# Attention, Fourier mixing and a gated convolution layer in fp32: two more products rounded for cheaper matmuls, another choice of added middle taps, and VectorE steps in another order

## The chip, the cores and the metric

The kernel runs on one core of one Trainium2 chip. The metric is the device time of one execution in microseconds (us), as a median over runs. All times below are in us.

## The reference, cut to what matters

Three layers follow each other on 4 batches of 1088 tokens with 128 channels. The first is a linear attention with product features, the second a Fourier mix over tokens and channels, a normalisation and a two-matmul layer (512 hidden channels), the third, where the change lies, is this one (1024 hidden channels, a convolution over tokens with three taps for each channel):

```python
def _moe2_ref(x, w_in, conv_w, w_out):
    h = np.maximum(x @ w_in, 0.0)
    hp = np.concatenate([zeros, h, zeros], axis=1)      # one token each side
    for k in range(3):
        conv_out += conv_w[k][None, None, :] * hp[:, k:k + S, :]
    gate = 1.0 / (1.0 + np.exp(-conv_out))
    return h * gate @ w_out
```

## The kernel before, in words

Channels lie on the 128 partitions, tokens in the free dimension. The second layer ("layer 1" in the change's words: normalised rows, w1, w2) is cut into ten units of four row tiles; a unit has four slots (one for each 128 of its 512 hidden channels), so there are 40 slots and two to finish them. The third layer is cut into 32 chunks, chunk i being batch i // 8 and the hidden channels i % 8 of 128. From chunk 0 on, both are interleaved by PACES: slots 23 to 41 are spread over the steps 0 to 22, in two places in each step (slots_a and slots_b).

In a step i TensorE does hidden(i) (L671, three matmuls of 364 tokens, each as three passes of a rounded number split into a high and a low half, L612), perhaps normed_transposes, slots, and project(n) (L686) of a chunk that lies LAGS steps back. A chunk runs through these instructions:

- relu (L894, ScalarE, three pieces) writes h2(i), a ring of HIDDENS = 5 buffers; relu(i) waits for product(i - 5).
- The left and the middle tap. Three ways: left_tap (L1177, VectorE) does both in one instruction. For chunks in ADDED, the left tap is a scaled copy on ScalarE (left_copy, L902) or, for those in SCALED, on VectorE (left_scaled, L1184), and the middle tap is an accumulating DMA from POOL's queue (add_middle, L474). An added chunk is "late": its right tap and all behind it come one step later.
- right_tap (L1190, VectorE), sigmoid (L911, ScalarE), product (L1199, VectorE; chunks 30 and 31 in three parts).
- project: plain, one fp32 matmul for each third of the tokens, which the trace shows as two records (L707), or, for chunks in CAST, "rounded": a DMA from POOL's queue casts the product to a rounded fp32 (cast_product, L483, three buffers, gate_hi, so that cast n waits for the project of the chunk three casts before), product_low (L1206, VectorE) takes what is left over, and the matmul is three passes.

Each engine works its list in order, written out by hand in the step loops: ScalarE's at L933, VectorE's at L1221, POOL's at L491, TensorE's at L754. Layer 1's low halves on VectorE are hidden_low (L1117), mixed_low (L1124) and normed_low (L1109); mixed_rows (L1072) adds the Fourier mix to a row set, moments and late_rows normalise. Slots 19 and 21 hold the normed_low of places 6 and 7, and the transposes of place 7 write the PSUM bank that the halves of place 6 are read from (L624). The adds and the casts alternate between two semaphores each, so that each waits for the one two before it.

The step loop of VectorE, in the order before:

```python
                for i in products_at(step):
                    product(i)
                if step + 1 in LAST_TURNS:
                    normed_low(LAST_TURNS[step + 1])
                for n in slots_a(step + 1):
                    slot(n)
                for i in rights(step):
                    right_tap(i)
```

Of the kernel before, what the change touches and what calls it, by code (L numbers as in the profile page):

```python
# [90 lines left out]
TURNS_AT = {2: 1, 6: 2, 10: 3, 14: 4, 17: 5, 19: 6, 21: 7}  # L91
# [2 lines left out]
PACES = ((0, 23), (30, 34), (46, 42))  # L94
HIDDENS = 5
VECTOR_ROWS = (8, 9)
ADDED = (4, 6, 7, 8, 9, 11, 12, 13, 15, 16, 17, 18, 20, 22, 24, 25, 26, 27, 28, 30)
CAST = (2, 4, 5, 6, 7, 11, 12, 13, 16, 17, 20, 21)
CASTS = 3
SCALED = (11, 17, 28)  # L100
ADDED_LATE, PRODUCT_AT, LOW_AT = 1, 2, 3
H2_PAD, H2_ROW = 15, 1120
GATES = 9
SPLIT_FROM = NI - 2
LAGS = ((-1, 7), (28, 6), (30, 5))
FINAL_LAG = LAGS[-1][1]
assert TQ * NJ == HALF and TT * NT == SP and TT % 2 == 0 and G1 % 2 == 0 and G1 <= 512

# [8 lines left out]
def build(nc, kT_d, qT_d, v_d, s_d, ident_d, chan_d, cos_d, sin_d, w1_d, w2_d, win_d, wout_d, cw_d, out_d):  # L117
    with ExitStack() as ctx:
# [143 lines left out]
        def bank_h1(n):  # L262
            return 2 + n % 3 if n < FIRST_SLOTS else 2
# [30 lines left out]
        def has_low(n):  # L294
            return n < LOW_UNTIL


        def products(i, t):
            return PRODUCT_ORDER.index(i) + 1 if i < SPLIT_FROM else SPLIT_FROM + NT * (i - SPLIT_FROM) + t + 1
# [5 lines left out]
        def gate(i):  # L305
            return attic[:, (i % GATES) * S:(i % GATES + 1) * S]


        def halves_free(n):

            return ((wout_done, NT * (CAST[n - CASTS] + 1)),) if n >= CASTS else ()


        def late(i):
            return ADDED_LATE if i in ADDED else 0


        COPIED = [i for i in ADDED if i not in SCALED]

        def rights(step):  # L320
            both = (step - ADDED_LATE, step) if step == NI - 1 else (step, step - ADDED_LATE)
            return [i for i in both if 0 <= i < NI and i + late(i) == step]
# [6 lines left out]
        def products_at(step):  # L329
            return [i for i in (step - PRODUCT_AT - ADDED_LATE, step - PRODUCT_AT) if 0 <= i < NI and i + PRODUCT_AT + late(i) == step]  # L330
# [18 lines left out]
        def slots_before(place):  # L349
            for (p0, n0), (p1, n1) in zip(PACES, PACES[1:]):  # L350
                if place <= p1:
                    return n0 + -(-(n1 - n0) * (place - p0) // (p1 - p0))
            return NC1 + 2
# [28 lines left out]
        def slots_b(i):  # L382
            return range(slots_before(2 * i + 1), slots_before(2 * i + 2))
# [50 lines left out]
        def _(pool):  # L434
# [39 lines left out]
            def add_middle(n, i):  # L474
                if i in SCALED:
                    pool.wait_ge(scaled, SCALED.index(i) + 1)
                else:
                    pool.wait_ge(copied, COPIED.index(i) + 1)
                if n >= 2:
                    pool.wait_ge(middle_added[n % 2], 16 * (n // 2))  # L480
                pool.dma_start(gate(i), h2(i)[:, 1:S + 1], accum_op=ALU.add).then_inc(middle_added[n % 2], 16)

            def cast_product(n, i):  # L483
                pool.wait_ge(prod_ready, products(i, 0))
                if n >= 2:
                    pool.wait_ge(cast_done[n % 2], 16 * (n // 2))
                for free, count in halves_free(n):
                    pool.wait_ge(free, count)
                pool.dma_start(gate_hi[:, n % CASTS, :], gate(i)).then_inc(cast_done[n % 2], 16)

            for step in STEPS:  # L491
                if step in ADDED:
                    add_middle(ADDED.index(step), step)
                for i in products_at(step):
                    if i in CAST:
                        cast_product(CAST.index(i), i)


        @block.tensor
        def _(pe):  # L500
# [185 lines left out]
            def project(i):  # L686
                b, c = divmod(i, C2)
                if i == 0:
                    pe.wait_ge(ld_wout, 32)
                n = CAST.index(i) if i in CAST else None  # L690
                if n == 0:
                    pe.wait_ge(wout_lo_ready, 1)
                if i in CAST:
                    pe.wait_ge(cast_done[n % 2], 16 * (n // 2 + 1))
                    pe.wait_ge(low_ready, n + 1)
                for t in range(NT):
                    if i not in CAST:
                        pe.wait_ge(prod_ready, products(i, t))
# [254 lines left out]
        def _(dve):  # L953
# [155 lines left out]
            def normed_low(r):  # L1109
                dve.wait_ge(unhi_ready, r + 1)  # L1110
                if 2 <= r < RING:
                    dve.wait_ge(w1_done, C1 * (r - 1))
                high, low = turned(r)
                dve.tensor_tensor(low, ps[:, bank_turned(r), 0:G1], high.bitcast(F32),  # L1114
                                  ALU.subtract).then_inc(unlo_ready, 1)

            def hidden_low(n):  # L1117
                dve.wait_ge(h1hi_ready, n + 1)
                if n >= 3:
                    dve.wait_ge(w2_done, n - 2)  # L1120
                dve.scalar_tensor_tensor(out=h1lo[:, n % 3, :], in0=ps[:, bank_h1(n), 0:G1], scalar=0.0,  # L1121
                                         in1=h1hi[:, n % 3, :].bitcast(F32), op0=ALU.max, op1=ALU.subtract).then_inc(h1lo_ready, 1)

            def mixed_low(r):  # L1124
                dve.wait_ge(x2hi_ready, written(r))
                for (turned, tokens), (_, high) in zip(token_views(x2lo, r), token_views(x2hi, r)):
                    dve.tensor_tensor(tokens, turned, high.bitcast(F32), ALU.subtract).then_inc(x2lo_ready, 1)  # L1127

            def slot(n):
                r, c = divmod(n, C1)  # L1130
                if n < NC1 and has_low(n):
                    hidden_low(n)
                if n in MIXED_AT:
                    mixed_rows(MIXED_AT[n])
                if c == 1 and r >= NJ:
                    mixed_low(r - 1)
                if n in MOMENTS_AT:
                    moments(MOMENTS_AT[n])
                if c == 2 and 1 <= r < NJ:
                    mixed_low(r - 1)  # L1140
                if n in TURNS_AT:
                    normed_low(TURNS_AT[n])
                if n in ROWS_AT and ROWS_AT[n] in VECTOR_ROWS:
                    late_rows(ROWS_AT[n])
# [45 lines left out]
            def right_tap(i):  # L1190
                if i in ADDED:
                    n = ADDED.index(i)
                    dve.wait_ge(middle_added[n % 2], 16 * (n // 2 + 1))
                else:
                    dve.wait_ge(left_ready, i - sum(n < i for n in ADDED) + 1)
                dve.scalar_tensor_tensor(out=gate(i), in0=h2(i)[:, 2:S + 2], scalar=ratio[:, 1, i % C2:i % C2 + 1],  # L1196
                                         in1=gate(i), op0=ALU.mult, op1=ALU.add).then_inc(conv_ready, 1)

            def product(i):  # L1199
                dve.wait_ge(gate_ready, SIGMOID_ORDER.index(i) + 1)  # L1200
                cuts = [t * TT for t in range(NT)] if i >= SPLIT_FROM else [0]
                for a, z in zip(cuts, cuts[1:] + [S]):
                    dve.tensor_tensor(gate(i)[:, a:z], h2(i)[:, 1 + a:1 + z], gate(i)[:, a:z],  # L1203
                                      ALU.mult).then_inc(prod_ready, 1)

            def product_low(n, i):  # L1206
                dve.wait_ge(cast_done[n % 2], 16 * (n // 2 + 1))
                dve.tensor_tensor(gate_lo[:, i % GATES, :], gate(i), gate_hi[:, n % CASTS, :].bitcast(F32),
                                  ALU.subtract).then_inc(low_ready, 1)
# [11 lines left out]
            for step in STEPS:  # L1221
                if step in SCALED:
                    left_scaled(step)
                elif step < NI and step not in ADDED:
                    left_tap(step)
                for i in products_at(step):
                    product(i)
                if step + 1 in LAST_TURNS:
                    normed_low(LAST_TURNS[step + 1])
                for n in slots_a(step + 1):  # L1230
                    slot(n)
                for i in rights(step):
                    right_tap(i)
                if step == 0:
                    late_rows(NR - 1)
                if step == 3:
                    wout_low()
                for n in slots_b(step + 1):
                    slot(n)
                for i in CAST:  # L1240
                    if i + LOW_AT + late(i) == step:
                        product_low(CAST.index(i), i)


def lag(i):

    return next(chunks for first, chunks in reversed(LAGS) if i >= first)

# [88 lines left out]
```

## Time and profile before

| | |
|---|---|
| median of 3 runs | 251.67 us (251.54 to 251.69) |
| the profiled execution | 252.02 us |
| its span, first to last instruction | 250.2 us |
| TensorE matmuls busy | 242.9 us, 97% |
| VectorE busy | 215.4 us, 86% |
| ScalarE busy | 170.8 us, 68% |
| granted TensorE clock | full in every slice |

The span is what the profile's times are counted in; 1.8 us of the execution lie around it. Matmuls are pipelined, so a matmul's duration is longer than the time it holds the engine, and the distance between two starts is what counts; the same holds, by a little, for VectorE and ScalarE. Idle time stands in square brackets behind an instruction, with the one that ended it.

### The profile page before, as it was taken

What the parts mean: (1) busy time and instruction counts of PE and PEld (TensorE: products, weight loads), DVE (VectorE), ACT (ScalarE), POOL (GpSimd) and SP (SyncE); (2) the same over time, 40 slices, a digit from 0 to 9 for tenths busy, and PEclk for the clock granted to TensorE, in tenths of its full rate; (3) what the DMA queues carried; (4) which work ended last, traced back from release to release, by engine and by line L of the source; (5) the groups of instructions that cost most, each with busy time, mean ns of one, the idle gap of its engine ahead of it and who ended that gap; (6) DMA issues with size and microseconds to landing.
All of it is one profiled execution on the core that took longest, in us unless ns stands there. A gap on an engine that the chain in (4) does not pass through costs nothing.

```text
span 250.2 us, 4440 instructions
## 1 busy us (share of the span) xinstructions
PE 242.9 (97%) x1558; PEld 215.1 (86%) x1558; DVE 215.4 (86%) x408; ACT 170.8 (68%) x334; POOL 53.3 (21%) x123
## 2 busy tenths in 40 slices
PE   8999999999999999998989999999999999999995
PEld 6999999999989998997978877998879879797753
DVE  0747888899998697899899999988969999989992
ACT  2452634332576566667799898999958989997852
POOL 0000000000624530665501332031421211321100
PEclk9999999999999999999999999999999999999999
DMA  6968830210000020000004799387988446997602
GB/s 194 392 243 320 344 101 3 62 40 0 3 0 0 4 84 1 3 3 3 0 0 89 186 261 217 141 165 195 262 206 158 135 134 181 280 196 157 170 3 89
DMA packets 9094, 31.41 MB, mean 126 GB/s; under 512 B 1264, under 2 KB 2032, under 8 KB 9072
## 3 DMA queue, kind: packets, MB, share of 16 engines
q0 software_dynamic: 4752, 18.35, 30.8%
q1 hardware_dynamic: 4176, 12.74, 14.1%
q8 instruction: 13, 0.21, 0.4%
q14 instruction: 9, 0.07, 0.1%
q10 hardware_dynamic: 144, 0.03, 0.1%
HBM read 10.54 MB, written 2.23 MB: 51 GB/s over the span
## 4 chain that ended last, share of the span: by engine, by line
PE 41%; DVE 11%; ACT 2%; issue 1%; ACTq 0%
PE ps L707 10%; PE ps L613 9%; PE ps L615 9%; PE ps L614 9%; PE ps L656 4%; DVE attic L1196 4%; DVE attic L1203 3%; DVE attic L1181 2%; DVE late_lo L1114 1%; PE ps L647 1%; ACT folded_room L900 1%; ACT arena L829 1%; DVE x2lo L1127 0%; ACT attic L915 0%; DVE wout_lo L1213 0%
## 5 line engine op out<-in xcount | busy, mean ns | idle before, releaser
L915 ACT ACTIVATE attic<-attic,base 128x1088 f32<-128x1088 f32 x32 | 37.9, 1204 | 4.6 <-DVE attic L1196 4.5
L707 PE MATMUL ps<-attic,wout 128*128 128x364 f32 (+1 forms) x120 | 39.1, 469 | 0.1
L613 PE MATMUL ps<-x2hi,wlo 128*128 128x364 f32 x96 | 37.2, 388 | 0.8 <-ACT folded_room L900 0.7
L707 PEld LDWEIGHTS ps<-attic,wout 128*128 128x128 f32 x120 | 22.5, 189 | 13.2 <-issue 2.1
L615 PE MATMUL ps<-x2hi,whi 128*128 128x364 f32 x96 | 31.6, 329 | 0.0
L614 PE MATMUL ps<-x2lo,whi 128*128 128x364 f32 x96 | 31.5, 328 | 0.0
L613 PEld LDWEIGHTS ps<-x2hi,wlo 128*128 128x128 f32 x96 | 18.1, 188 | 4.9 <-ACT folded_room L900 1.7
L900 ACT ACTIVATE x_room<-ps 128x364 f32<-128x364 f32 x42 | 18.3, 479 | 4.0 <-PE ps L615 3.7
L458 POOL TENSOR_SCALAR arena<-arena 109x4 f32<-109x4 f32 x10 | 2.0, 197 | 88.4 <-DVE arena L1099 88.3
L1196 DVE SCALAR_TENSOR_TENSOR attic<-x_room,ratio,attic 128x1088 f32<-128x1088 f32 x14 | 18.7, 1348 | 1.7 <-DMA attic<-x_room 1.6
L614 PEld LDWEIGHTS ps<-x2lo,whi 128*128 128x128 f32 x96 | 18.1, 188 | 2.4 <-issue 1.1
L780 ACT ACTIVATE attic<-ps 109x320 f32<-109x320 f32 (+2 forms) x16 | 6.7, 425 | 18.4 <-PE ps L528 16.1
L540 PE MATMUL ps<-attic 121*128 121x66 f32 x144 | 18.6, 270 | 0.0
L1203 DVE TENSOR_TENSOR attic<-x_room,attic 128x1088 f32<-128x1088 f32 (+2 forms) x18 | 18.1, 1035 | 0.4 <-ACT attic L915 0.4
L900 ACT ACTIVATE folded_room<-ps 128x364 f32<-128x364 f32 x36 | 15.3, 477 | 4.1 <-PE ps L615 3.9
L615 PEld LDWEIGHTS ps<-x2hi,whi 128*128 128x128 f32 x96 | 18.0, 188 | 0.0
L1121 DVE SCALAR_TENSOR_TENSOR h1lo<-ps,h1hi 128x436 fp32r<-128x436 f32 x22 | 13.2, 605 | 5.5 <-ACT h1hi L843 5.5
L540 PEld LDWEIGHTS ps<-attic 121*128 121x128 f32 x144 | 17.7, 192 | 0.0
L571 PE MATMUL ps<-arena 128*109 128x66 f32 x160 | 17.1, 260 | 0.1
L528 PE MATMUL ps<-sketch,attic 128*109 128x64 f32 (+1 forms) x152 | 17.1, 267 | 0.0
L788 ACT ACTIVATE arena<-ps 128x436 f32<-128x436 f32 x20 | 10.6, 534 | 9.3 <-PE ps L555 9.2
L528 PEld LDWEIGHTS ps<-sketch,attic 128*109 128x109 f32 (+1 forms) x152 | 16.7, 185 | 0.2
(130 smaller groups left out, 621.6 us busy)
## 6 DMA issues: line engine op xcount, KB each, us to landing
gate_hi<-attic POOLq DMA_DIRECT2D x12, 544.0 KB, 3.5
attic<-folded_room POOLq DMA_DIRECT2D x9, 544.0 KB, 5.0
attic<-x_room POOLq DMA_DIRECT2D x8, 544.0 KB, 5.3
attic<-v_d SPq DMA_DIRECT2D x4, 594.0 KB, 3.8
attic<-qT_d SPq DMA_DIRECT2D x3, 545.0 KB, 7.0
attic<-kT_d SPq DMA_DIRECT2D x3, 544.5 KB, 6.1
attic<-arena POOLq DMA_DIRECT2D x3, 544.0 KB, 5.3
out_d<-arena SPq DMA_DIRECT2D x3, 544.0 KB, 4.7
```

The source lines that it names most:

```text
L528: mm = pe.matmul(ps[0:rows, bank_kq(n), c:c + H * AB], src[:, b % 2, t * rows:(t + 1) * rows], sketch[:], start=True, stop=True)
L540: mm = pe.matmul(ps[:, KV_BANK, pair * 2 * V1:(pair + 1) * 2 * V1], kphi[:, b % 2, t, 2 * pair:2 * pair + 2, :].rearrange("p h f -> p (h f)"),
L571: mm = pe.matmul(ps[0:TQ, bank, c:c + 2 * V1], qphiT[:, 2 * t + pair, :], kvz[:, pair, :], start=True, stop=True)
L613: pe.matmul(out, lo, rhi, start=first, stop=False)
L614: pe.matmul(out, hi, rlo, start=False, stop=False)
L615: return pe.matmul(out, hi, rhi, start=False, stop=last)
L707: pe.matmul(ps[:, OUT_BANK + t, 0:z - a], wout[:, c, :], gate(i)[:, a:z], start=(c == 0), stop=(c == C2 - 1)).then_inc(wout_done, 1)
L900: act.activation(h2(i)[:, t * TT:(t + 1) * TT], ps[:, bank_p(n), 0:TT], ACT.Relu).then_inc(h2_ready, 1)
L915: act.activation(gate(i), gate(i), ACT.Sigmoid, scale=base[:, i % C2:i % C2 + 1]).then_inc(gate_ready, 1)
L1121: dve.scalar_tensor_tensor(out=h1lo[:, n % 3, :], in0=ps[:, bank_h1(n), 0:G1], scalar=0.0, in1=h1hi[:, n % 3, :].bitcast(F32), op0=ALU.max ...
L1196: dve.scalar_tensor_tensor(out=gate(i), in0=h2(i)[:, 2:S + 2], scalar=ratio[:, 1, i % C2:i % C2 + 1], in1=gate(i), op0=ALU.mult, op1=ALU.a ...
L1203: dve.tensor_tensor(gate(i)[:, a:z], h2(i)[:, 1 + a:1 + z], gate(i)[:, a:z], ALU.mult).then_inc(prod_ready, 1)
```

## The change

It does five things.

- CAST gets the chunks 3 and 8: 14 rounded projections, not 12.
- ADDED loses 8 and 27 and gets 10 (19, not 20); SCALED loses 28, which stays added and gets its scaled copy on ScalarE. 8 and 27 become left taps.
- LAGS: project stays 7 steps behind up to step 28 and is 6 behind from 29 on (before: 7, 6 from 28, 5 from 30). So the projections come in the order 21 | 22, 23 | 24 | 25 in the steps 28 to 31, and 26 to 31 behind the last step (before 21, 22 | 23 | 24, 25 | 26, and 27 to 31).
- In VectorE's step loop the right taps come ahead of the late normed_low and of slots_a; the lows of the rounded products come ahead of slots_b.
- In slot 19 the normed_low of place 6 comes ahead of mixed_rows.

```diff
-ADDED = (4, 6, 7, 8, 9, 11, 12, 13, 15, 16, 17, 18, 20, 22, 24, 25, 26, 27, 28, 30)
-CAST = (2, 4, 5, 6, 7, 11, 12, 13, 16, 17, 20, 21)
+ADDED = (4, 6, 7, 9, 10, 11, 12, 13, 15, 16, 17, 18, 20, 22, 24, 25, 26, 28, 30)
+CAST = (2, 3, 4, 5, 6, 7, 8, 11, 12, 13, 16, 17, 20, 21)
 CASTS = 3
-SCALED = (11, 17, 28)
+SCALED = (11, 17)
...
-LAGS = ((-1, 7), (28, 6), (30, 5))
+LAGS = ((-1, 7), (29, 6))
...
                 if n < NC1 and has_low(n):
                     hidden_low(n)
+                if n in TURNS_AT and n == 19:
+                    normed_low(TURNS_AT[n])
                 if n in MIXED_AT:
                     mixed_rows(MIXED_AT[n])
...
-                if n in TURNS_AT:
+                if n in TURNS_AT and not n == 19:
                     normed_low(TURNS_AT[n])
...
                 for i in products_at(step):
                     product(i)
+                for i in rights(step):
+                    right_tap(i)
                 if step + 1 in LAST_TURNS:
                     normed_low(LAST_TURNS[step + 1])
                 for n in slots_a(step + 1):
                     slot(n)
-                for i in rights(step):
-                    right_tap(i)
                 if step == 0:
                     late_rows(NR - 1)
                 if step == 3:
                     wout_low()
-                for n in slots_b(step + 1):
-                    slot(n)
                 for i in CAST:
                     if i + LOW_AT + late(i) == step:
                         product_low(CAST.index(i), i)
+                for n in slots_b(step + 1):
+                    slot(n)
```

## Rows read from the trace of the kernel before

**Rows 1.** The page's first part: busy time, share and instructions of each engine.

```profile
PE 242.9 (97%) x1558; PEld 215.1 (86%) x1558; DVE 215.4 (86%) x408; ACT 170.8 (68%) x334; POOL 53.3 (21%) x123
```

**Rows 2.** Busy by stretches: PE, PEld, DVE, ACT, POOL, then clock, DMA share, GB/s.

```profile
139.00:157.00 18.00, 17.87 (x85) 14.25 (x85) 17.27 (x18) 15.65 (x30) 5.14 (x7) 1.00 0.96 245
...
240.00:250.20 10.20, 7.29 (x24) 3.95 (x22) 5.65 (x9) 3.83 (x5) 0.00 (x0) 1.00 0.16 56
```

**Rows 3.** The chain that ended last: start, length, engine and line.

```profile
140.33 2.54 DVE attic L1196 x2
...
145.60 0.43 PE ps L613
...
152.05 1.83 PE ps L707 x6
...
235.89 0.18 PE ps L615
...
242.89 0.55 DVE attic L1203
...
243.48 3.94 PE ps L707 x12
```

**Rows 4.** TensorE's timeline: start, length, line and operation, operands, idle before.

```profile
114.82 0.56 PE L626 MATMUL ps<-ident,arena 109*128 109x109 f32 x4 [1.03 <-DVE late_lo L1114]
...
116.81 0.39 PE L613 MATMUL ps<-x2hi,wlo 128*128 128x364 f32 x1
...
147.20 0.33 PE L613 MATMUL ps<-gate_hi,wout_lo 128*128 128x364 f32 x1
...
148.68 0.36 PE L613 MATMUL ps<-late_hi,wlo 128*128 128x436 f32 x1
...
158.05 0.33 PE L613 MATMUL ps<-x2hi,wlo 128*128 128x364 f32 x1
```

**Rows 5.** VectorE's timeline.

```profile
112.74 0.48 DVE L1081 TENSOR_TENSOR arena<-ps,arena 109x130 f32<-109x130 f32 x2
...
114.08 0.60 DVE L1114 TENSOR_TENSOR late_lo<-ps,late_hi 128x436 fp32r<-128x436 f32 x1
...
115.64 0.67 DVE L1127 TENSOR_TENSOR x2lo<-ps,x2hi 128x218 fp32r<-128x218 f32 x2
...
122.56 1.12 DVE L1106 TENSOR_SCALAR arena<-x_room,arena 109x128 f32<-109x128 f32 x4 [0.65 <-POOL arena L472]
...
143.14 1.29 DVE L1208 TENSOR_TENSOR gate_lo<-attic,gate_hi 128x1088 fp32r<-128x1088 f32 x1 [0.28 <-DMA gate_hi<-attic]
...
147.28 0.74 DVE L1127 TENSOR_TENSOR x2lo<-ps,x2hi 128x218 fp32r<-128x218 f32 x3 [0.44 <-ACT x2hi L848]
...
152.86 1.29 DVE L1203 TENSOR_TENSOR attic<-x_room,attic 128x1088 f32<-128x1088 f32 x1
154.06 1.35 DVE L1196 SCALAR_TENSOR_TENSOR attic<-folded_room,ratio,attic 128x1088 f32<-128x1088 f32 x1
155.33 1.35 DVE L1181 SCALAR_TENSOR_TENSOR attic<-x_room,ratio 128x1088 f32<-128x1088 f32 x1
...
161.52 0.79 DVE L1188 TENSOR_SCALAR attic<-x_room,ratio 128x1088 f32<-128x1088 f32 x1
```

**Rows 6.** ScalarE's timeline.

```profile
112.05 1.66 ACT L829 ACTIVATE arena<-x_room,arena 109x128 f32<-109x128 f32 x4
...
145.09 1.18 ACT L900 ACTIVATE folded_room<-ps 128x364 f32<-128x364 f32 x3
```

**Rows 7.** POOL's timeline.

```profile
119.36 1.21 POOL L466 TENSOR_TENSOR arena<-arena 109x4 f32<-109x4 f32 x1
...
138.17 0.56 POOL L489 DMA_DIRECT2D gate_hi<-attic  x1 [4.13 <-DVE attic L1203]
```

**Rows 8.** The lines L489 (12 casts) and L481 (20 adds): from issue to landing.

```profile
DMA to landing us min/median/max: 2.9/3.5/5.0
...
DMA to landing us min/median/max: 4.6/5.2/7.4
```

## The prediction

> **What bounds the kernel now.** I read the page's busy shares first: TensorE's matmul side is busy 97% of the span [rows 1]. So a gain must come either from fewer or cheaper matmul instructions, or from the few places where TensorE stands still. Next the table by stretches: in 139 to 157 us VectorE is busy 17.27 of 18 us and the 16 DMA engines 96%, at the full granted clock; at the end TensorE is busy 7.29 of 10.2 us, and most of what is missing there is the tail behind its last matmul [rows 2]. Then the chain that ended last. It shows three kinds of place: a wait for VectorE before 114.8 us, a VectorE-ScalarE-TensorE hand-over up to 145.60, and from there TensorE without a break until 235.89 plus its own width; after that the last chunk's VectorE work, and TensorE again at 243.48 [rows 3]. Timelines of the single engines give the sizes:
>
> - In the gap before the transposes of place 7, TensorE sat idle for 1.03 until 114.82, waiting for the low half that VectorE finished at 114.68 [rows 4, 5].
> - At 145.60 hidden(9) follows project(1): it waited for the relu of chunk 8 that started at 145.09, itself behind two sigmoids that waited for the right taps of 5 and 4 (140.33) [rows 3, 6].
> - At the end, four plain projections of 1.83 fill 235.89 to 243.21, and product(30), from 242.89 on, lets the next start at 243.48: 0.27 lost [rows 3].
>
> I call left, right, product, low the VectorE work on a chunk (L1181, L1196, L1203, L1208). By starts in a row without idle, a product or low takes 1.20 and a tap 1.26 (152.86, 154.06, 155.33) [rows 5].
>
> **Step 1: the low half of place 6 ahead of mixed rows 9.** It now starts at 114.08, behind 1.34 of mixed rows; it will start at 112.74 and end at 113.34. The next thing the transposes need is the scaled rows, which ScalarE finishes at 112.05 + 1.66 = 113.71 [rows 5, 6]. So TensorE goes on at about 113.85, 0.97 earlier. Not all of it is kept. Nothing behind both VectorE pieces moves: their sum is the same. hidden(0), at 116.81 now, needs the second part of the low half at 115.64, done at 116.31: it starts at about 116.4, 0.4 earlier [rows 4, 5]. The mixed rows end 0.52 later, hidden by the h1 low halves, which start at 114.60 as before. From here VectorE's own queue decides up to 145.6, and its idle time there (0.65 at 122.56, and a smaller wait for the low half of place 8, which the right tap of 1, now ahead of it, fills) gives back what it can [rows 5]. I take 0.36 at 145.60; the ends are 0.1 (only the relu of chunk 0 a bit earlier) and 0.4 (all that hidden(0) has gained). The late half of place 9 starts 1.2 later, cover: its reader, slot 28, comes after hidden(6).
>
> **Step 2: chunks 3 and 8 rounded.** A plain projection is six records and 1.83; a rounded one is nine, 147.20 to 148.68 = 1.48 [rows 3, 4]. That is 0.35 less on TensorE for each, 0.70 together. VectorE gets two lows, 2.40; POOL two casts, the DMA engines two transfers. Nothing else of the dtype changes.
>
> **Step 3: the middle taps.** 8 and 27 go from a ScalarE copy and an accumulating DMA to a left tap, 10 the other way, 28 from a VectorE scaling (0.79) to a ScalarE copy. VectorE: +1.26 three steps early in the crowded stretch (chunk 8), -1.26 at 10, +0.56 net at 27/28 (1.35 - 0.79) [rows 5]. The DMA engines lose one add.
>
> **Where steps 2 and 3 meet: relu(11).** The hidden values lie in a ring of five, so relu(11) waits for product(6), and hidden(12), at 158.05 now, waits for relu(11) [rows 4]. From low(2) at 143.14 to product(6) at 152.86 VectorE now spends 9.72. After the change low(3) (1.20), left(8) (1.26) and right(8) (1.26, one step earlier, since 8 is no longer late) stand ahead of product(6) too; right(6) ahead of slot 29 fills the idle 0.44 at 147.28 [rows 5]. 9.72 + 3.72 - 0.44 = 13.00. low(2) starts at 143.14 - 0.36 = 142.78, product(6) at 155.78, ends at 157.07; relu(11) at 157.1; hidden(12) 0.51 after it, as 145.09 to 145.60 now [rows 3, 6]: 157.6, 0.45 before its place now. TensorE by itself would be 0.36 + 0.35 = 0.71 ahead. So here VectorE, not TensorE, sets the pace, and every wait in its queue before 155.8 counts in full.
>
> **The unknown: when cast 3 lands.** product(3) ends about 139.97, its cast can be issued at about 140.3, and low(3)'s turn is 143.98. Casts take 2.9 to 5.0 to land, median 3.5; the one issued at 138.17 just ahead took the 5.0 [rows 7, 8]. So the wait of low(3) lies between 0 (2.9 and 3.5) and 1.3 (5.0). A longer one isn't excluded: add(6) now comes right behind cast 3 on POOL, and adds take 4.6 to 7.4 [rows 8]. I take 4.0, nearer to the median: 0.3 of wait. The POOL queue is also held by the ring of three rounded halves: cast 5 now waits for project(2), 148.68 (its low's turn is after 154), cast 8 for project(5), with add(11) behind it; add(10) is queued behind cast 6, at about 158.3, and right(10)'s turn is 163, with a landing of 5.2 a wait of 0.5. product(9) then ends about 168.4, and relu(14), which waits for it, may start up to 169.1 before hidden(15) moves. Cost taken: 0, bounds 0 and 0.6.
>
> A row speaks against this: at 119.36 a 0.20 us POOL operation took 1.21 and ended 0.05 after VectorE's tap [rows 7]. The Trainium skill (SBUF — State Buffer, the trap "DVE blocks DMA") says that GpSimd can't write the descriptors of its DMA while certain VectorE instructions hold the port pair that both share. By that rule a cast might wait one further tap, 1.35, and the sum below would end at about +0.5; against it, the issue instruction of the cast at 138.17 took 0.56, and VectorE was busy then too, so the landing times above hold what there is of it [rows 7].
>
> **Step 4: right taps ahead of slots, lows ahead of slots, the lag.** Only slots 25, 29, 33, 37, 41 have VectorE work; the lows' move changes no order at all, the right taps' move steps 7, 17 and 21. Slot 29's low halves, needed by a transpose three records behind 148.68, about 149.3, end by 149.0 to 149.8: 0 to 0.4 of stall, taken as 0. With the lag, project(25) comes behind hidden(31): seven chunks behind it, not six, so the last hidden chunk comes 1.83 earlier and VectorE has 1.83 more for the tail, against +0.56 of step 3. The sigmoid of 26, behind the output copies on ScalarE, costs it some 0.6 by my walk through the order. product(30) then starts at 242.89 - 1.83 - 0.50 + 0.56 + 0.6 = 241.7 (0.50 is what TensorE has gained by then). Its first part, 0.55, is due at 243.21 - 0.50, so it may start up to 242.2 [rows 3]: the 0.27 wait goes, and some 0.03 more in the last split parts. Taken: 0.30, bounds 0 and 0.38.
>
> **Sum.** hidden(12): -0.45 + 0.3 = -0.15. project(8): -0.35. End: -0.30. Together -0.80. The profiled execution took 252.02 (span 250.2); it would take 251.2. It stands 0.35 above the median of the runs, 251.67, and I subtract from that: 250.9.
>
> **The rivals.**
> - Cast 3 lands as its neighbour does (5.0): -0.45 + 1.3 - 0.65 = +0.2, 251.9. For it: DMA engines at 96%, an add right behind. Against: most casts were faster. 0.22.
> - Slower: low(3) is held as adds are. Place: VectorE at 144 us, everything behind it up to relu(11). At 6.3 (between 5.2 and 7.4) the wait is 2.6: +1.5, 253.2. It decides from a landing of about 5.3 on (+0.5). The rule above pulls this way. 0.11.
> - TensorE's own limit: no cast wait, and VectorE catches up: -0.36 - 0.70 - 0.30 = -1.36, 250.3. For it: a landing of 3.5. Against: the 13.00 of VectorE work. 0.15.
> - The reorder doesn't do what it is said to: TensorE at 114 us is held by the rows from ScalarE or VectorE's queue gives nothing back, so 0.36 is 0: -0.44, 251.2. 0.10.
> - The forecast: 0.42.
>
> **The numbers.** A measurement of this kernel tells 0.2%, 0.5 us, from no change. Faster by more: forecast 0.42, limit 0.15, and 0.06 of the fourth rival: 0.63. Within: 0.22 + 0.04: 0.26. Slower: 0.11. The range 250.2 to 252.2 takes in -1.4 (limit) and +0.5 (cast landing at 5.3); it leaves out the slower rival.
>
> **What would show it.** TensorE's gap at 114.8 down to some 0.2; rounded projections at 1.48 for chunks 3 and 8; product(6) at about 156.1, VectorE waiting some 0.3 for cast 3, and hidden(12) at 157.9; a gap of some 0.5 in TensorE right before it; no wait before product(30)'s projection. The forecast is wrong if hidden(12) isn't earlier than 158.05, if low(3) waits over 1 us, or if a new wait stands behind 170 us, where I count none.

## The result, and the profile after

The changed kernel is slower: 252.71 us, median of 12 runs, against 252.01 of 12 of the kernel before on the same chip. Some executions of most kernels here, before too, take 33 us more, all of it ahead of hidden(0) where a trace shows one (e2, e4, f2, h3: hidden(0) at 149.5 to 149.8, otherwise 115.9 to 117.2), so they are left out of the table's medians and of the ratios, and the stretches of those four stand in brackets. By the 11 and 10 executions that are left the medians are 252.59 and 251.84, and the ratio is 1.0032, with a 95% interval of 1.0021 to 1.0042, so 0.8 us. The forecast was 250.9. The profiled execution took 252.48 with a span of 250.7, against 252.02 and 250.2: of the 0.8 the trace shows some 0.5.

The page's busy shares, after, answer to [rows 1]: VectorE has 3.2 us more work.

```profile
PE 243.1 (97%) x1564; PEld 216.2 (86%) x1564; DVE 218.6 (87%) x410; ACT 170.0 (68%) x334; POOL 53.7 (21%) x124
```

The table by stretches, columns as in [rows 2]:

```profile
139.00:157.00 18.00, 17.49 (x87) 14.29 (x86) 17.96 (x18) 15.51 (x27) 4.38 (x6) 1.00 0.82 218
...
240.00:250.70 10.70, 7.90 (x26) 4.58 (x25) 5.99 (x9) 3.83 (x5) 0.00 (x0) 1.00 0.14 52
```

Between 139 and 157 us VectorE is busy 17.96 of 18.00 us: nothing is left there. TensorE lost 0.38 of its 17.87.

TensorE's timeline of the changed kernel, which answers to [rows 4]:

```profile
113.82 0.59 PE L626 MATMUL ps<-ident,arena 109*128 109x109 f32 x4
...
116.88 0.40 PE L613 MATMUL ps<-x2hi,wlo 128*128 128x364 f32 x1 [0.63 <-DVE x2lo L1127]
...
149.93 0.56 PE L647 MATMUL ps<-ident,x_room 109*128 109x109 f32 x4 [0.45 <-DVE x2lo L1127]
...
170.72 0.44 PE L613 MATMUL ps<-x2hi,wlo 128*128 128x364 f32 x1 [0.51 <-ACT arena L900]
```

The gap of 1.03 at 114.82 is gone, but a gap of 0.63 stands ahead of hidden(0), which starts at 116.88, not at 116.4. And there are two new gaps: at slot 29's transposes, 149.93, and ahead of hidden(15), 170.72.

VectorE's timeline (left L1183, scaled L1190, right L1198, product L1205, low L1210), which answers to [rows 5]:

```profile
115.71 0.67 DVE L1127 TENSOR_TENSOR x2lo<-ps,x2hi 128x218 fp32r<-128x218 f32 x2
...
142.88 2.59 DVE L1210 TENSOR_TENSOR gate_lo<-attic,gate_hi 128x1088 fp32r<-128x1088 f32 x2
145.38 1.28 DVE L1205 TENSOR_TENSOR attic<-arena,attic 128x1088 f32<-128x1088 f32 x1
...
147.79 1.35 DVE L1198 SCALAR_TENSOR_TENSOR attic<-x_room,ratio,attic 128x1088 f32<-128x1088 f32 x1
149.05 0.73 DVE L1127 TENSOR_TENSOR x2lo<-ps,x2hi 128x218 fp32r<-128x218 f32 x3
...
156.01 1.28 DVE L1205 TENSOR_TENSOR attic<-x_room,attic 128x1088 f32<-128x1088 f32 x1
...
163.44 1.35 DVE L1198 SCALAR_TENSOR_TENSOR attic<-x_room,ratio,attic 128x1088 f32<-128x1088 f32 x1 [0.58 <-DMA attic<-x_room]
...
167.60 1.29 DVE L1210 TENSOR_TENSOR gate_lo<-attic,gate_hi 128x1088 fp32r<-128x1088 f32 x1 [1.43 <-DMA gate_hi<-attic]
168.81 1.28 DVE L1205 TENSOR_TENSOR attic<-arena,attic 128x1088 f32<-128x1088 f32 x1
```

The two lows at 142.88 are low(2) and low(3), with no wait. Low(8), at 167.60, waited 1.43 for its cast. The casts and adds on POOL, by the DMA-issuing instructions of L489 and L481:

```profile
157.59 0.55 POOL L489 DMA_DIRECT2D gate_hi<-attic  x1 [6.66 <-DVE attic L1205]
158.12 0.92 POOL L481 DMA_DIRECT2D attic<-x_room  x1
159.15 0.55 POOL L489 DMA_DIRECT2D gate_hi<-attic  x1
163.45 0.53 POOL L489 DMA_DIRECT2D gate_hi<-attic  x1 [3.76 <-PE ps L615]
```

These are cast 6, add 10, cast 7 and cast 8. Cast 8 is held until project(5) has read its half. The chain that ended last goes through it, and at the end it has no step of VectorE any more:

```profile
163.45 4.12 DMA gate_hi<-attic
167.60 1.29 DVE gate_lo L1210
168.90 1.21 DVE attic L1205
170.19 0.48 ACT arena L900
170.72 0.44 PE ps L613
...
235.10 12.81 PE ps L707 x42
```

**Where the time went.** I measure a stretch, from the start of the second record of hidden(9) to the end of TensorE's last matmul, since the start of the whole shifts a little from one execution to the next. Before, that is 247.42 - 145.87 = 101.55; after, 247.91 - 145.88 = 102.03. By the second records of the hidden chunks, and counted from that of hidden(9), it divides into: hidden(10) 0.68 later (slot 29's gap); project(3), between hidden(10) and hidden(11), 4.65 to 4.36, so -0.29; hidden(15) a further 0.77 later (1.16 in all; its first record is at 170.72); project(8), between hidden(15) and hidden(16), 5.04 to 4.75, so -0.29; and the end -0.39. Together +0.48. The table gives this stretch for each kernel. It is one execution each: two of the changed kernel, this one and h3, differ by 0.19, so stretches that are closer than 0.2 can't be told apart. The ratio isn't the quotient of the two medians beside it (for g2 that is 0.9973, for g3 0.9975, for h2 0.9964); differences of 0.1% are not to be read.

| kernel | what differs | median us | before, same chip | ratio (95%) | stretch us |
|---|---|---|---|---|---|
| before | | 251.84 | | 1 | 101.55 |
| changed | | 252.59 | 251.84 | 1.0032 (1.0021 to 1.0042) | 102.03 |
| e1 | right(6) behind slot 29 | 252.1, 252.83 | 251.91 | none (two runs) | 101.83 |
| e2 | chunk 8 plain | 251.75 | 251.91 | 0.9988 (0.9977 to 0.9999) | (101.34) |
| e3 | both of these | 251.50 | 251.91 | 0.9982 (0.9969 to 0.9995) | 101.10 |
| e4 | slot 19's order as before | 252.86 | 251.91 | 1.0036 (1.0024 to 1.0049) | (102.74) |
| f1 | low(8) a step later | 253.42 | 251.94 | 1.0057 (1.0035 to 1.0078) | 102.89 |
| f2 | f1 and e1 | 253.63 | 251.94 | 1.0053 (1.0028 to 1.0079) | (102.98) |
| f3 | e3, lag as before | 251.74 | 251.94 | 0.9991 (0.9977 to 1.0006) | 102.00 |
| f4 | chunk 3 plain | 251.55 | 251.94 | 0.9981 (0.9966 to 0.9995) | 100.98 |
| g1 | e1, low(8) behind slot 33 | 254.25 | 252.09 | 1.0069 (1.0048 to 1.0089) | 102.75 |
| g2 | chunks 3 and 8 plain | 251.41 | 252.09 | 0.9965 (0.9952 to 0.9978) | 101.20 |
| g3 | the kernel before, new lag | 251.45 | 252.09 | 0.9967 (0.9955 to 0.9979) | 101.15 |
| g4 | add 10 ahead of cast 6 | 252.03 | 252.09 | 0.9994 (0.9979 to 1.0008) | 101.79 |
| h1 | g4 and e1 | 251.91 | 251.96 | 0.9996 (0.9979 to 1.0013) | 101.50 |
| h2 | g4 and f4 | 251.06 | 251.96 | 0.9959 (0.9943 to 0.9975) | 100.90 |
| h3 | the changed kernel again | 252.83 | 251.96 | 1.0038 (1.0015 to 1.0060) | (101.84) |

All edits are made to the changed kernel, but for g3.

### The profile page after: what moved, and what is told of

Same layout as the page of the kernel before. It is cut to its first block, busy times and chain, and to the rows that moved or that the text cites. A ratio compares the mean times of both kernels' runs of the same rounds, so it can differ in the third digit from the quotient of the medians.

```text
span 250.7 us, 4455 instructions
## 1 busy us (share of the span) xinstructions
PE 243.1 (97%) x1564; PEld 216.2 (86%) x1564; DVE 218.6 (87%) x410; ACT 170.0 (68%) x334; POOL 53.7 (21%) x124
## 4 chain that ended last, share of the span: by engine, by line
PE 36%; DVE 14%; POOL 2%; DMA 2%; issue 1%; ACT 1%; POOLq 0%; ACTq 0%
PE ps L707 12%; PE ps L613 7%; PE ps L615 7%; PE ps L614 7%; DVE attic L1205 3%; PE ps L656 3%; DVE attic L1198 3%; DVE attic L1183 2%; DMA gate_hi<-attic 2%; DVE gate_lo L1210 2%; DVE x2lo L1127 1%; DVE late_lo L1114 1%; DVE arena L1093 1%; PE ps L647 1%; POOL arena L468 1%
## 5 line engine op out<-in xcount | busy, mean ns | idle before, releaser
L707 PE MATMUL ps<-attic,wout 128*128 128x364 f32 (+1 forms) x108 | 34.7, 468 | 0.0
L707 PEld LDWEIGHTS ps<-attic,wout 128*128 128x128 f32 x108 | 20.4, 190 | 11.7 <-issue 1.6
L1210 DVE TENSOR_TENSOR gate_lo<-attic,gate_hi 128x1088 fp32r<-128x1088 f32 x14 | 18.0, 1288 | 2.2 <-DMA gate_hi<-attic 2.1
L1198 DVE SCALAR_TENSOR_TENSOR attic<-x_room,ratio,attic 128x1088 f32<-128x1088 f32 x14 | 18.7, 1349 | 0.9 <-DMA attic<-x_room 0.8
L1205 DVE TENSOR_TENSOR attic<-x_room,attic 128x1088 f32<-128x1088 f32 (+2 forms) x18 | 18.1, 1034 | 0.4 <-ACT attic L915 0.2
L489 POOL DMA_DIRECT2D gate_hi<-attic x14 | 7.7, 549 | 44.2 <-DVE attic L1205 32.8
```

What stands on the lines that cost most here:

```text
L707: pe.matmul(ps[:, OUT_BANK + t, 0:z - a], wout[:, c, :], gate(i)[:, a:z], start=(c == 0), stop=(c == C2 - 1)).then_inc(wout_done, 1)
```

## The experiments

### The two new gaps, each undone

e1 puts right(6) back behind slot 29, as before:

```diff
-                for i in rights(step):
+                for i in rights(step) if step != 7 else ():
                     right_tap(i)
...
                 for n in slots_a(step + 1):
                     slot(n)
+                for i in rights(step) if step == 7 else ():
+                    right_tap(i)
```

> The changed kernel, but in step 7 the right tap of 6 comes behind slot 29 again, as before the change. Theory (two separate new stalls): TensorE's 0.45 us gap ahead of the transposes at 149.9 goes, hidden(10) is back near 150.6, and since cast 8 waits for project(5) it is issued 0.6 earlier too, so hidden(15) and the end come 0.6 earlier: 0.9975 of the changed kernel, about 252.1. Rival (VectorE simply has more work than fits, and sets the pace wherever it is asked): right(6), left(8) and the lows move back by the 0.44 of idle that slot 29 then costs, product(6) is at 156.4, and the end moves by less than 0.2 us.

Measured: TensorE's timeline of e1 at the two places:

```profile
149.14 0.54 PE L647 MATMUL ps<-ident,x_room 109*128 109x109 f32 x4
...
170.28 0.43 PE L613 MATMUL ps<-x2hi,wlo 128*128 128x364 f32 x1 [0.85 <-ACT arena L900]
```

So with right(6) behind slot 29 the gap there goes, and hidden(10) comes 0.65 earlier (counted from hidden(9)). But the gap ahead of hidden(15) grew from 0.51 to 0.85, and at hidden(15) only 0.27 was left: cast 8 was issued 0.6 earlier and took 4.5 to land, not 4.1. The stretch fell by 0.20, no more than two executions of one kernel differ by, and its two runs, 252.10 and 252.83, leave open whether the kernel is faster at all.

e2 leaves chunk 8 plain, by its cast:

```diff
-CAST = (2, 3, 4, 5, 6, 7, 8, 11, 12, 13, 16, 17, 20, 21)
+CAST = (2, 3, 4, 5, 6, 7, 11, 12, 13, 16, 17, 20, 21)
```

> The changed kernel with chunk 8's projection plain again (13 rounded). Theory: the gap at 149.9 stays; low(8) with its 1.43 us wait for a cast that waited for project(5) is gone, product(9) ends near 167.5, the gap of 0.5 ahead of hidden(15) goes (0.8 us earlier), project(8) costs 0.35 more: 0.4 us faster than the changed kernel, about 252.3. Rival (more work than fits): hidden(15) is earlier by less than 0.35 and the kernel is no faster than the changed one.

Measured: 0.9988 against 1.0032, so 1.1 us less than the changed kernel although project(8) costs 0.29 more again. Its trace has no gap ahead of hidden(15), and one of 0.30 at slot 29. e3 is e1 and e2 in one.

> Both of the two edits before. Theory: 0.6 + 0.4 = 1.0 us less than the changed kernel, so 0.996 of it and 0.2 us or more below the kernel before (0.999): neither gap is in the trace. Rival: a third wait takes their place between 150 and 175 us and the sum is under 0.5.

Measured: 0.9982, stretch 101.10. TensorE's timeline of e3 shows neither gap:

```profile
149.03 0.54 PE L647 MATMUL ps<-ident,x_room 109*128 109x109 f32 x4
...
169.36 0.33 PE L613 MATMUL ps<-x2hi,wlo 128*128 128x364 f32 x1
```

With both mended the stretch falls by 0.93 from 102.03, with e1's edit alone by 0.20. By the runs e3 (0.9982) can't be told from e2 (0.9988): nearly all of the gain comes with chunk 8, and what slot 29's order adds to it isn't shown by them.

### Slot 19 as before

e4 undoes the edit in slot 19 (the low half of place 6 behind mixed rows 9 again):

```diff
-                if n in TURNS_AT and n == 19:
-                    normed_low(TURNS_AT[n])
...
-                if n in TURNS_AT and not n == 19:
+                if n in TURNS_AT:
```

> The changed kernel with slot 19 in its old order. Theory: hidden(0) is set by the second low half of unit 4 (VectorE, ends 116.38, 0.5 us ahead of the matmul) in either order, so the 1.0 us gap comes back at 114.8 and the 0.63 us gap at 116.9 goes; hidden(0) and the end stay within 0.1 us: same time as the changed kernel. Rival: the order gave part of what was forecast (0.36) and its loss is masked, then this kernel is 0.1 to 0.2% slower than the changed one.

Measured: 1.0036 against 1.0032 for the changed kernel. The edit gives nothing that shows. Its trace has TensorE's gap of 1.03 ahead of the transposes again and none ahead of hidden(0), as the theory said; g3 below, which also lacks the edit, has a gap of 1.00 at 115.09 and loses nothing by it.

### Low(8) later in VectorE's queue: a theory that fell

Low(8) waits 1.43 for its cast and product(9) stands behind it. I held that moving low(8) a step later would let product(9), relu(14) and hidden(15) go. f1:

```diff
-                    if i + LOW_AT + late(i) == step:
+                    if i + LOW_AT + late(i) + (i == 8) == step:
```

> The changed kernel, with the low half of product 8 one step later on VectorE, behind product(9) and right(11): the same work, the same cast, only nothing queued behind the wait but what follows right(11). Theory (the wait in the queue costs, not the work): product(9) starts near 166.2 instead of 168.8, the gap of 0.51 ahead of hidden(15) goes, and the end comes 0.8 us earlier with the 0.35 of project(8) kept: 0.997 of the changed kernel, about equal to the kernel before (1.000). Rival (VectorE's total of work): the 1.20 of the low half is only moved to before right(12), the stall shows up at hidden(16) or (17), and the kernel stays at 1.003 of the one before.

Measured: slower, 1.0057. VectorE's timeline of f1:

```profile
166.21 1.28 DVE L1205 TENSOR_TENSOR attic<-arena,attic 128x1088 f32<-128x1088 f32 x1
...
170.53 1.35 DVE L1198 SCALAR_TENSOR_TENSOR attic<-x_room,ratio,attic 128x1088 f32<-128x1088 f32 x1 [3.03 <-DMA attic<-x_room]
171.79 1.29 DVE L1210 TENSOR_TENSOR gate_lo<-attic,gate_hi 128x1088 fp32r<-128x1088 f32 x1
173.00 0.67 DVE L1127 TENSOR_TENSOR x2lo<-ps,x2hi 128x218 fp32r<-128x218 f32 x2
```

and TensorE's:

```profile
173.82 0.56 PE L647 MATMUL ps<-ident,x_room 109*128 109x109 f32 x4 [1.27 <-DVE x2lo L1127]
```

Product(9) came 2.6 earlier, as expected, and it was worth nothing: the next in the queue, right(11), then waited 3.03 for add 11, with low(8) behind it and slot 33's low halves behind that, and TensorE stood still for 1.27 there. Low(8) had been filling a wait that would have been there without it: in the changed kernel right(11) starts at 170.15, behind product(9).

f2 adds e1's edit to it.

> The same, and in step 7 slot 29 ahead of the right tap of 6. Theory: both new gaps of TensorE (149.9 and 170.7) are gone and both cheap projections are kept: 0.35 us less than the run that had slot 29 first and chunk 8 plain (0.9982 of the kernel before), so 0.997, a span of about 249.2, with cast and ring costs taken as nil. Rival: cast 8 (held for project(5)) still delays add 11, right(11) waits for it some 0.5 us or more, and nothing is won over the plain chunk 8.

Measured: 1.0053, no better than f1. In its trace slot 29's gap is gone, right(11) waits 3.10 and the gap ahead of slot 33's transposes is 1.84. g1 tried the last place left, behind slot 33:

```diff
-                    if i + LOW_AT + late(i) == step:
+                    if i + LOW_AT + late(i) == step and i != 8:
...
                 for n in slots_b(step + 1):
                     slot(n)
+                if step == 12:
+                    product_low(CAST.index(8), 8)
```

> The changed kernel with slot 29 ahead of right(6) and the low half of product 8 in step 12, now behind slot 33. Theory: the 1.27 us gap at 173.8, which the first try (ahead of slot 33) opened since slot 33's low halves stood behind low(8), is gone, and so are those at 149.9 and ahead of hidden(15), but for what relu(14) waits behind the sigmoid of 10. By starts from hidden(9) to the last matmul 101.1 (before 101.53, changed 102.02), some 0.998 of the kernel before. Rival: VectorE's total is too much, a new gap of over 0.5 opens behind 173, and the kernel is no faster than 1.001.

Measured: 1.0069, the slowest. The wait for add 11 was still there, in VectorE's timeline of g1:

```profile
169.26 1.35 DVE L1198 SCALAR_TENSOR_TENSOR attic<-x_room,ratio,attic 128x1088 f32<-128x1088 f32 x1 [2.85 <-DMA attic<-x_room]
```

Its profiled execution was also its fastest, 252.24 against a median of 254.25, so the trace (a gap of 0.31 at 171.35, one of 0.72 at 209.05, ahead of hidden(24)) shows only a part of the loss.

### The lag, taken back and by itself

f3 is e3 with the lags of before:

```diff
-LAGS = ((-1, 7), (29, 6))
+LAGS = ((-1, 7), (28, 6), (30, 5))
```

> The run with slot 29 first and chunk 8 plain (span 249.5, 0.9982 of the kernel before), with the old lags (7, 6 from step 28, 5 from 30). Theory: the lag gives VectorE 1.83 us more for the tail; without it product(30) is late by 0.4 to 1.0 us more than its slot, and the gap ahead of the last two projections comes back: 0.3 to 0.8 us slower, 0.9995 to 1.001 of the kernel before. Rival: the tail has slack anyway once VectorE is early, and nothing changes (under 0.1).

Measured: 0.9991 against 0.9982 of e3. The chain of f3 has the wait for product(30) again:

```profile
242.79 0.55 DVE attic L1205
243.38 3.94 PE ps L707 x12
```

The stretch rose by 0.90, more than the end explains. The rest is in the middle of this execution: low(2) waited 0.52 for a cast that took 5.2 to land, and relu(11), behind product(6), came late, as TensorE's timeline of f3 shows:

```profile
157.85 0.43 PE L613 MATMUL ps<-x2hi,wlo 128*128 128x364 f32 x1 [0.48 <-ACT x_room L900]
```

That is the gap that I had forecast for the changed kernel, and here it came with a late landing.

g3 is the other way round, the kernel before with the new lag and nothing else (the same two lines of the diff, reversed).

> The kernel before with the new lags alone. Theory: the 0.27 us wait for product(30) and some 0.1 in the last parts go, nothing else moves: 0.3 to 0.4 us less, 0.9987. Rival: output copies and sigmoids of ScalarE stand in the tail, product(30) is late again, and it is 1.000.

Measured: 0.9967, stretch 101.15, 0.40 less than before; the ratio stands for 0.8 us, the two medians for 0.6, and what the runs have above the trace stays open. TensorE's tail in the chain is one piece:

```profile
234.42 12.81 PE ps L707 x42
```

g2 is the changed kernel with chunks 3 and 8 both plain; taps, orders and lag stay changed:

```diff
-CAST = (2, 3, 4, 5, 6, 7, 8, 11, 12, 13, 16, 17, 20, 21)
+CAST = (2, 4, 5, 6, 7, 11, 12, 13, 16, 17, 20, 21)
```

> The changed kernel with only the 12 rounded chunks of before (taps, order and lag as changed). Theory: no low(3) and no low(8), so no gap at 149.9 and none ahead of hidden(15); the taps and the order cost nothing, the lag gives 0.38 at the end: hidden(9) to the last matmul 101.15 (before 101.53), 0.9985 of the kernel before, that is, rounding 3 and 8 is all of the changed kernel's loss and 0.7 of TensorE's work is not won. Rival: the earlier left and right tap of 8 (2.5 us of VectorE) hold product(6) and relu(11), a gap stays ahead of hidden(12), and it is 1.000 or more.

Measured: 0.9965, stretch 101.20. It is g3's time within the error: the middle taps and the three reorders together give nothing that these runs can tell, the lag gives the gain, and the two rounded projections make all of the loss. In the stretch their price is 102.03 - 101.20 = +0.83; the two profiled executions, 252.48 and 251.35, are 1.13 apart, the other 0.3 lying ahead of hidden(9). By the runs it is more: (1.0032 - 0.9965) x 252 = 1.7 us, or 1.4 by the medians. What makes up the rest stays open. Other gaps that come and go may be part of it: g1's of 0.72 ahead of hidden(24), or one of 0.30 ahead of the last two projections in the trace of e4, which has the new lag.

### Chunk 3 plain, and the add ahead of the cast

f4 leaves chunk 3 plain instead of 8:

```diff
-CAST = (2, 3, 4, 5, 6, 7, 8, 11, 12, 13, 16, 17, 20, 21)
+CAST = (2, 4, 5, 6, 7, 8, 11, 12, 13, 16, 17, 20, 21)
```

> The changed kernel with chunk 3 plain again (13 rounded, 8 among them). Theory: low(3)'s 1.20 on VectorE is what put slot 29's low halves behind the transposes: without it they end near 148.7 and the gap at 149.9 (0.6 by starts) goes, at the price of 0.35 for project(3); cast 8 is still held by project(5) and the wait ahead of product(9) stays. Net 0.2 to 0.3 us faster than the changed kernel, about 1.002 of the kernel before. Rival: the gap stays, since right(6) alone holds slot 29, and the kernel is 0.35 slower.

Measured: 0.9981, stretch 100.98, a larger gain than I had expected. In VectorE's timeline of f4 slot 29's low halves come 0.92 earlier, though hidden(9) is 0.32 later in this execution:

```profile
148.13 0.73 DVE L1127 TENSOR_TENSOR x2lo<-ps,x2hi 128x218 fp32r<-128x218 f32 x3
```

and TensorE's has neither gap, with chunk 8 still rounded:

```profile
149.60 0.54 PE L647 MATMUL ps<-ident,x_room 109*128 109x109 f32 x4
...
170.00 0.43 PE L613 MATMUL ps<-x2hi,wlo 128*128 128x364 f32 x1
```

(By the second records hidden(15) is 0.14 later behind hidden(14) than before, 3.14 for 3.00.) Right(6) stands ahead of slot 29 here as in the changed kernel, so its place alone doesn't make the gap: right(6) and low(3) together do, and taking away either closes it. Without the 1.20 of low(3), product(6), cast 6 and add 10 are all 1.2 earlier, counted from hidden(9), and cast 8 landed 3.5 after its issue, not 4.1. So one extra low in this queue is carried, and two are not. By the runs f4 and e3 (0.9981, 0.9982) are no better than g2 (0.9965), although their stretches are shorter by 0.22 and 0.10: one rounded chunk more is worth nothing that can be told from noise.

Add 10 had been in flight beside cast 8. g4 issues it a step earlier, ahead of cast 6:

```diff
-                if step in ADDED:
+                if step in ADDED and step != 10:
...
+                if step == 9:
+                    add_middle(ADDED.index(10), 10)
```

> The changed kernel with add 10 ahead of cast 6 in POOL's queue (its copy is done at 154.5, cast 6 waits for product(6), 157.3). Theory (cast 8 lands late because cast 6 holds add 10, whose transfer then shares the DMA engines with casts 7 and 8): add 10 lands near 160 instead of 163.4, right(10) doesn't wait (0.58), cast 8, still issued behind project(5) at 163.5, lands in 3 instead of 4.12, low(8) waits 0.9 less, hidden(15) comes 0.7 to 0.8 earlier: 1.000 to 1.001 of the kernel before. Rival (project(5) holds cast 8, and that alone counts): its landing stays above 167.2, the gain is under 0.4.

Measured: 0.9994, stretch 101.79. The casts and add 10 on POOL in g4 (its lines behind the edit are two further than the changed kernel's):

```profile
154.99 0.88 POOL L481 DMA_DIRECT2D attic<-x_room  x1 [4.32 <-ACT attic L910]
157.81 0.55 POOL L489 DMA_DIRECT2D gate_hi<-attic  x1 [1.94 <-DVE attic L1207]
...
163.66 0.53 POOL L489 DMA_DIRECT2D gate_hi<-attic  x1 [3.77 <-PE ps L617]
```

Cast 8 landed 3.2 after its issue, cast 7 too (5.7 in the changed kernel), and low(8) started at 166.83, in VectorE's timeline of g4:

```profile
166.83 1.29 DVE L1212 TENSOR_TENSOR gate_lo<-attic,gate_hi 128x1088 fp32r<-128x1088 f32 x1 [1.29 <-DMA gate_hi<-attic]
```

So 0.78 was gained at hidden(15), which had no gap. But slot 29's gap was larger in this execution:

```profile
150.14 0.56 PE L649 MATMUL ps<-ident,x_room 109*128 109x109 f32 x4 [0.93 <-DVE x2lo L1129]
```

Nothing ahead of it was edited. Cast 2 landed 5.1 after its issue here, and low(2) waited for it, in VectorE's timeline of g4:

```profile
143.10 2.58 DVE L1212 TENSOR_TENSOR gate_lo<-attic,gate_hi 128x1088 fp32r<-128x1088 f32 x2 [0.46 <-DMA gate_hi<-attic]
```

In the changed kernel cast 2 took 4.7, low(2) had no wait, and the gap was 0.45; in f1 4.6 and 0.40. The 0.46 of wait is about what g4's gap has above those two. h1 adds e1's edit:

> The changed kernel with slot 29 ahead of right(6) and add 10 ahead of cast 6: both new gaps' causes mended, both chunks rounded. Theory (two gaps, each with a cause of its own: the order at slot 29, and the DMA transfers behind add 10): from hidden(9) to the last matmul 100.6 to 100.9 (before 101.53, changed 102.02), 0.995 to 0.997 of the kernel before. Rival (low(3) and the casts' landing hold VectorE in any case): a gap of 0.3 us or more stays ahead of hidden(12) or (15), and it is no better than the lag alone (0.9967).

Measured: 0.9996, stretch 101.50. Slot 29 has no gap, but cast 8 took 4.1 to land this time, so low(8) waited 1.88 and a gap of 0.53 stands ahead of hidden(15):

```profile
166.72 1.29 DVE L1212 TENSOR_TENSOR gate_lo<-attic,gate_hi 128x1088 fp32r<-128x1088 f32 x1 [1.88 <-DMA gate_hi<-attic]
```

The order of the adds doesn't settle when cast 8 lands. h2 joins g4 and f4:

> The changed kernel with chunk 3 plain and add 10 ahead of cast 6. Theory: nothing is left of either gap, project(8) and the lag give 0.35 + 0.38: hidden(9) to the last matmul 100.8, 0.996 of the kernel before. Rival: right(11) or low(8) waits still hold product(9) by 0.3 or more, and it equals the run with chunk 3 plain alone (0.9981).

Measured: 0.9959 (0.9943 to 0.9975), stretch 100.90: faster than both kernels, by 1.0 us (0.9 by the medians) over before. Low(8) still waits 1.39, but it starts earlier, at 165.56, there is room behind it, and hidden(15) has no gap, in TensorE's timeline of h2:

```profile
169.17 0.33 PE L615 MATMUL ps<-x2hi,wlo 128*128 128x364 f32 x1
```

By its interval it can't be told from g2 and g3.

h3 ran the changed kernel once more.

> The changed kernel once more, beside the two above. Theory (its gap at 149.9 hangs on when casts 2 and 3 land, which differs from execution to execution): the gap there is between 0.4 and 1.0 us, and its size goes with the start of product(4) on VectorE; the ratio is 1.003 again. Rival: the gap is the same 0.45 whatever the casts do.

Measured: 1.0038 (1.0015 to 1.0060), which repeats the result of the change. In its trace the gap at slot 29 is 0.27, with a cast 2 that took 4.3, and the one ahead of hidden(15) 0.56. So neither the rival's fixed 0.45 nor the theory's 0.4 to 1.0 holds, but the size does go with cast 2: 4.3 and 0.27, 4.6 and 0.40, 4.7 and 0.45, 5.1 and 0.93 (h3, f1, changed, g4).

## Why the prediction was wrong

The terms that I had added up were hidden(12) -0.15, project(8) -0.35 and the end -0.30. Measured, counted from hidden(9), they are +0.35, -0.29 and -0.39, and from hidden(12) to hidden(15) stands another +0.81 (0.77 from hidden(11)), for which I had put nothing: together +0.48. Of the distance between 250.9 and 252.71, another 0.3 is the base: I started from a median of three runs, 251.67, and twelve gave 252.01. Two of my own signs of being wrong came: hidden(12), at 158.41, isn't earlier than 158.05, and a new wait stands behind 170 us.

- **Step 1 failed in its bound for hidden(0).** "It starts at about 116.4" took only the operand's end (116.31) as the limit. The traces show 0.5 between the end of that VectorE work and the matmul in both kernels: 116.31 to 116.81 before, 116.38 to 116.88 after (0.36 to 0.52 over all the kernels here). TensorE wasn't idle in that interval before, so no wait showed in [rows 4], and I took it for a start in turn. The 1.00 gained at the transposes (114.82 to 113.82) was returned whole, hidden(9) is at 145.61 against 145.60, and the 0.36 is 0. The fourth rival was right that the 0.36 is 0, though not by its mechanism at 114 us (the transposes did come at 113.82, as I had put it), and its time of 251.2 was wrong with mine.
- **Cast 3 and product(6) were right.** Low(3) waited 0 (I took 0.3; its cast landed in 3.5), product(6) started at 156.01 (forecast 156.1). The rival that low(3) is held, mine for a slower kernel, didn't come about. Relu(11) didn't hold hidden(12) either: it started at 157.52, directly behind two sigmoids on ScalarE, and hidden(12) at 158.41 in its turn, since TensorE was later by then than I had it.
- **Step 4's term for slot 29 failed.** I bounded it by 0 and 0.4 and took 0. It measured 0.45 of idle time, and 0.68 by hidden(10)'s start. The low halves ended at 149.05 + 0.73 = 149.78, the late end of my own 149.0 to 149.8, against 149.3 needed. From low(2)'s start, 142.88, two lows, two products and right(6) at their own lengths give 142.88 + 2.40 + 2.40 + 1.26 = 148.94, and 0.73 more 149.67, with no wait in it: the rows spoke for the late end, and I took the early one. The matmuls were also 0.15 behind their operand (149.78 to 149.93). e1, without right(6) in front of the slot, and f4, without low(3), both have no gap: it takes the two together.
- **The POOL-queue term failed.** "Cost taken: 0, bounds 0 and 0.6": it measured 0.77 at hidden(15). I had held product(9) to end at about 168.4; it started only at 168.81. What I had not priced is low(8)'s own wait. I had seen that cast 8 is held by project(5), but then counted only right(10)'s wait of 0.5 (measured: 0.58). Issue at 163.45 and a landing of 4.12 put low(8) at 167.60, 1.43 idle, and low(8) and one product behind it make relu(14) 170.19 - 169.1 = 1.1 later than the limit that I had given.
- **The saving of a rounded projection was 0.29 by starts, not 0.35** (0.28 to 0.34 in the other kernels), and **the end was right**: its VectorE wait is gone, -0.39 against -0.30, and g3 shows it alone.
- **The rule on GpSimd's descriptors did not decide.** All the issue instructions of the casts took 0.53 to 0.56, with VectorE busy 17.96 of 18 us. The Trainium skill (SBUF — State Buffer, the trap "DVE blocks DMA") states the block for VectorE operations in a 2-port performance mode; that a tap is one was my assumption, which no row showed, and a wait of one tap per cast isn't seen in the issue instructions. The landings, 2.9 to 5.7, could hold some of it, and no run here separates that.

The slower outcome, to which I gave 0.11 through one mechanism at 144 us, came through another one, at 149 and 164 us, from the same source: two more lows, and two more casts to wait for, in a VectorE queue that had no idle time left to pay for them. g2 against the changed kernel shows that by taking away the two lows and casts alone; it keeps the earlier tap of chunk 8 and has neither gap.

**What stays open:** why landings of the same cast differ by over 1 us (cast 8: 4.1 in the changed kernel, 4.5 in e1, 3.5 in f4, 3.2 in g4, 4.1 in h1, 3.0 in h2), why the loss by the runs (1.4 to 1.7 us against g2) is larger than that of the profiled executions (1.13), and what passes in the 0.5 us between x2lo and hidden(0). The low and the cast of a chunk were never taken apart, so how much of the price is VectorE's 1.20 and how much the wait for the landing is told by the traces, not by an experiment.

## What to carry to other kernels

When one engine is busy nearly all of a stretch (VectorE 17.27 of 18 us here), price work added to it at its full duration at every deadline behind it, with the deadlines in order; a stall that is mended there can come back at the next one, as in e1 and f1. For each DMA whose issue is held by a buffer, work out issue plus landing at both ends of the landing times, and compare it with its reader's turn: one of them, low(8)'s, was the largest term (0.77) and I never wrote it down. When a change has several parts, the cheapest of them (here one line, the lag) may hold all of the gain that can be measured, so run it by itself.

## What the runs showed of the hardware that was not expected

- The landing of one and the same cast (128 x 1088, cast in SBUF) went from 2.9 to 5.7 us in the changed kernel, median 3.9, against 2.9 to 5.0 and 3.5 before [rows 8]; adds from 4.6 to 8.2. The long ones stand behind others: cast 7, right behind add 10, took 5.7, and add 12, behind cast 8 and add 11, took 8.2.
- For cast 7 the order decides. In the changed kernel, e1, e3, f1, f3, f4, g1 and g2 it is issued 0.7 to 2.0 us behind add 10, takes 4.7 to 6.1 and lands 1.3 to 1.5 after the add, however far apart the two were issued. In g4, h1 and h2, which are the changed kernel, e1 and f4 with add 10 ahead of cast 6 and nothing else, it takes 3.2, 3.2 and 2.9 (5.7, 6.0 and 4.8 without). For cast 8 no such rule comes out: 3.2 in g4, but 4.1 in h1 with the same order.
- A wait need not show as idle time: 0.5 us passed between VectorE's end and hidden(0)'s start both before, when TensorE had other work, and after, when it stood idle. It isn't a constant: e1 and g1 had 0.36.
